# The first MLP product by Strassen's scheme, in groups of six tiles

## The reference

```python
attn = softmax(mask(q @ k^T / 8)) @ v          # 4 x 8 heads, 576 x 64, window of 64
x = attn as (2304, 512)
x[do] = x[do] + gate * (relu(x[do] @ w1[e]) @ w2[e])   # MoE: one of 8 experts for each row that computes
h = x @ w_in                                   # (2304, 512) @ (512, 2048)
g = h * clip(h + 3, 0, 6) / 6
out = g @ w_out                                # (2304, 2048) @ (2048, 512)
```

## Time and profile before

| | us |
|---|---|
| median of three runs | 698.57 (698.03 to 699.78) |
| the profiled execution, its own time | 699.17 |
| its span, first to last instruction | 697.6 |
| TensorE busy in it | 659.5 |
| VectorE, ScalarE, GpSimd busy | 251.9, 243.1, 71.9 |

### The profile page before, as it was taken

One profiled execution on the slowest core, in us unless ns is written; L12 is line 12 of the kernel. 1 busy time (PEld: TensorE's weight loads), 2 busy tenths in 40 slices (PEclk: granted clock), 3 DMA queues, 4 the chain that ended last, 5 costly groups with the idle time before them and its releaser, 6 DMA issues.

```text
span 697.6 us, 17145 instructions
## 1 busy us (share of the span) xinstructions
PE 659.5 (95%) x6654; PEld 580.8 (83%) x6654; DVE 251.9 (36%) x810; ACT 243.1 (35%) x571; POOL 71.9 (10%) x122
## 2 busy tenths in 40 slices
PE   5799997679999999899999999999999999999998
PEld 4678886658877887899899989998999899989996
DVE  2568886001111112465442224223422242233222
ACT  3779984011121112465432223222322232223221
POOL 4322564111111111000000000000000000000000
PEclk9999998899999999999999999999999999999999
DMA  9767879788486176453220002000200020001001
GB/s 171 148 151 194 218 210 388 239 307 292 156 304 219 36 274 194 140 169 121 91 91 0 1 2 90 0 0 0 90 0 0 0 90 0 0 0 47 0 1 45
DMA packets 97155, 78.13 MB, mean 112 GB/s; under 512 B 61697, under 2 KB 76805, under 8 KB 97104
## 3 DMA queue, kind: packets, MB, share of 16 engines
q1 hardware_dynamic: 81632, 44.88, 23.6%
q10 hardware_dynamic: 12496, 26.24, 11.0%
q0 software_dynamic: 2976, 6.32, 2.7%
HBM read 63.23 MB, written 17.52 MB: 116 GB/s over the span
## 4 chain that ended last, share of the span: by engine, by line
PE 81%; DMA 7%; DVE 4%; SPq 3%; ACT 2%; issue 2%; POOLq 0%; DVEq 0%; ACTq 0%
PE bank L844 29%; PE bank L857 19%; PE av L857 10%; PE av L818 7%; PE bank L806 6%; DMA xin<-x_rows 6%; PE bank L619 2%; PE av L663 2%; DVE sm L1081 2%; SPq L412 2%; PE bank L679 2%; PE bank L604 1%; PE av L775 1%; ACT pr L903 1%; PE av L829 1%
## 5 line engine op out<-in xcount | busy, mean ns | idle before, releaser
L1027 ACT ACTIVATE rel<-bank,half 128x384 f32<-128x384 f32 x96 | 55.8, 582 | 185.5 <-PE bank L844 185.5
L1279 DVE SCALAR_TENSOR_TENSOR act<-rel,bank 128x384 f32<-128x384 f32 x96 | 53.2, 554 | 170.1 <-ACT rel L1027 170.1
L844 PE MATMUL bank<-xT_hi,wi_hi 128*128 128x384 f32 x384 | 83.3, 338 | 0.7 <-ACT xT_hi L1020 0.7
L844 PE MATMUL bank<-xT_hi,wi_lo 128*128 128x384 f32 x384 | 82.8, 336 | 0.0
L844 PE MATMUL bank<-xT_lo,wi_hi 128*128 128x384 f32 x384 | 82.0, 334 | 0.0
L1283 DVE TENSOR_TENSOR g_lo<-act,g_hi 128x384 fp32r<-128x384 f32 x96 | 53.6, 558 | 66.8 <-ACT g_hi L1038 66.8
L857 PE MATMUL bank<-wo_hi,g_lo 128*128 128x512 f32 x192 | 76.1, 397 | 0.0
L857 PE MATMUL bank<-wo_hi,g_hi 128*128 128x512 f32 x192 | 76.0, 396 | 0.0
L857 PE MATMUL bank<-wo_lo,g_hi 128*128 128x512 f32 x192 | 75.7, 394 | 0.0
L844 PEld LDWEIGHTS bank<-xT_hi,wi_hi 128*128 128x128 f32 x384 | 68.9, 188 | 7.7 <-ACT xT_hi L1020 0.9
L1038 ACT CAST g_hi<-act 128x384 fp32r<-128x384 f32 x96 | 49.3, 513 | 64.8 <-DVE act L1279 64.8
(11 more groups left out here) (139 smaller groups left out, 794.4 us busy)
## 6 DMA issues: line engine op xcount, KB each, us to landing
w2s<-in_moe_w ACTq DMA_DIRECT2D x7, 2048.0 KB, 10.9
w1s<-in_moe_w ACTq DMA_DIRECT2D x5, 2048.0 KB, 15.9
qraw<-in_q SPq DMA_DIRECT2D x36, 128.0 KB
vnow<-in_v SPq DMA_DIRECT2D x36, 128.0 KB, 3.4
x_new<-xall SPq DMA_DIRECT2D x18, 256.0 KB
out<-ot SPq DMA_DIRECT2D x18, 256.0 KB, 2.1
kraw<-in_k SPq DMA_DIRECT2D x34, 128.0 KB
xn<-x_new SPq DMA_DIRECT2D x17, 256.0 KB, 3.3
```

Source lines behind the costliest of these rows:

```text
L844: last = pe.matmul(bank[f % 4][:, 0:GN], a[:, f, c, :], b[:, c, :], start=(n == 0), stop=(n == 3 * DC - 1))
L1027: sc.activation(rel[f % 2][:, :], bank[f % 4][:, 0:GN], ACT.Relu, scale=1.0 / 6.0, bias=half[:, :]).then_inc(s_rel, 1)
L1279: dve.scalar_tensor_tensor(out=act[f % 2][:, :], in0=rel[f % 2][:, :], scalar=1.0, in1=bank[f % 4][:, 0:GN], op0=ALU.min, op1=ALU.mult).th ...
```

## The change

Six tiles form a group (three groups), and two units form a pair (eight pairs). For a group and a pair, the first product is a 2 by 2 by 2 block product: the 512 inputs are halved (`k`), the six tiles are halved (`t`), and the pair has two units (`u`). Strassen's scheme (in a form with 7 products) computes the four blocks of h from seven products of sums of quarters instead of eight products of quarters.

- **x**: for each group, ScalarE copies the six turned tiles to `xr`. VectorE (three) and GpSimd (two) form five sums or differences of quarters in the buffers `xd[0]` and `xd[1]`, and two quarters are used as they are. ScalarE rounds each of the seven (`x_high`), and VectorE takes the rest (`x_low`).
- **weights**: they are no longer kept. For each group and pair SyncE loads a piece of each weight, GpSimd forms five sums (`combine_w`), and ScalarE and VectorE split them (`w_high`, `w_sums_high`, `w_low`, `o_high`, `o_low`).
- **products**: `product(it, j)` is 6 matmuls of 384 columns into bank 6 or 7 by turns. ScalarE copies products 0 to 4 to SBUF (`mc`). GpSimd forms two blocks of h and two part sums (`hq`, `tsum`, `usum`). VectorE adds products 5 and 6 to the part sums from PSUM. Then relu, act, g_hi and g_lo as before, with two of the four g_lo on GpSimd.
- **second product**: its 36 matmuls for six tiles and two units stand between the products of the next iteration, into banks 0 to 5. The next group's tiles are turned at the end of the iterations 1 to 6 of a group.

The buffers move too: `xc_hi`, `xc_lo`, `xr`, `rel` and `act` lie where the experts' weights were, and the first group's tiles 3 to 5 are loaded into the buffers `ot`. The loops of the MLP are written out in full and no longer run as device loops.

The diff, cut to the parts above:

```diff
-    GN = GT * P
-    NRAW = 4
+    MT = 6
+    MG = NT // MT
+    FP = FC2 // 2
+    NQ = MG * FP
+    GN = MT // 2 * P
+    XQ = DC // 2
...
+        PIECES = ((0, 0), (0, 1)), ((0, 2), (1, 0)), ((1, 1), (1, 2)), ((2, 0), (2, 1)), ((2, 2), (3, 0)), ((3, 1),), ((3, 2),)
+        def m_bank(j):
+            return bank[6 + j % 2]
...
+        def turned(it):
+            G, p = it // FP + 1, it % FP
+            return (G, p - 1) if G < MG and 1 <= p <= MT else None
...
+            def load_w_in(it):
+                if it >= 2:
+                    sp.wait_ge(s_wlo, it - 1)
...
+                for u in range(2):
+                    for h in range(2):
+                        sp.dma_start(wir[it % 2][:, 1 - u + 2 * h, :, :], quarters[:, u, it % FP, h, :, :]).then_inc(s_wir[it % 2], 16)
...
+            def combine_w(it):
+                w, lot = wir[it % 2], wcm
+                pool.wait_ge(s_wir[it % 2], 64 * (it // 2 + 1))
+                if it:
+                    pool.wait_ge(s_wlo, it)
+                pool.tensor_tensor(lot[:, 0:2, :, :], w[:, 0:2, :, :], w[:, 2:4, :, :], ALU.add)
+                pool.tensor_tensor(lot[:, 2:4, :, :], w[:, 0:4:3, :, :], w[:, 1:3, :, :], ALU.subtract)
+                pool.tensor_tensor(lot[:, 4, :, :], w[:, 1, :, :], w[:, 2, :, :], ALU.add).then_inc(s_wcm, 1)
...
+            combine_w(0)
+            combine_x(0, 4)
+            combine_x(0, 6)
+            for it in range(NQ):
+                last_pair = it % FP == FP - 1 and it + 1 < NQ
+                if it + 1 < NQ:
+                    combine_w(it + 1)
+                pool.wait_ge(s_hq, 5 * it + 2)
+                if it:
+                    pool.wait_ge(s_act, 4 * it - 3)
+                pool.tensor_tensor(hq[0][:, :], mc[0][:, :], mc[1][:, :], ALU.add).then_inc(s_cp, 1)
+                pool.wait_ge(s_hq, 5 * it + 3)
+                if it:
+                    pool.wait_ge(s_mc, 2 * it - 1)
+                pool.tensor_tensor(tsum[:, :], mc[1][:, :], mc[2][:, :], ALU.subtract).then_inc(s_cp, 1)
+                if last_pair:
+                    combine_x(it // FP + 1, 4)
+                pool.wait_ge(s_hq, 5 * it + 4)
+                if it:
+                    pool.wait_ge(s_act, 4 * it - 2)
+                pool.tensor_tensor(hq[1][:, :], mc[3][:, :], mc[2][:, :], ALU.add).then_inc(s_cp, 1)
+                if it:
+                    pool.wait_ge(s_mc, 2 * it)
+                pool.tensor_tensor(usum[:, :], mc[3][:, :], mc[0][:, :], ALU.subtract).then_inc(s_cp, 1)
+                low(it, 0)
+                pool.wait_ge(s_hq, 5 * it + 5)
+                pool.wait_ge(s_cp, 6 * it + 4)
+                pool.tensor_tensor(tsum[:, :], tsum[:, :], mc[4][:, :], ALU.add).then_inc(s_cp, 1)
+                pool.tensor_tensor(usum[:, :], usum[:, :], mc[4][:, :], ALU.add).then_inc(s_cp, 1)
+                low(it, 1)
+                if last_pair:
+                    combine_x(it // FP + 1, 6)
...
+            def product(it, j):
+                G, p = it // FP, it % FP
+                if j == 0:
+                    pe.wait_ge(s_wlo, it + 1)
+                    if it:
+                        pe.wait_ge(s_mc, 2 * it)
+                elif j == 1:
+                    if it and turned(it - 1):
+                        pe.wait_ge(s_xr, turned(it - 1)[0] * MT + turned(it - 1)[1] + 1)
+                else:
+                    pe.wait_ge(s_hq, 5 * it + j - 1)
+                if p == 0:
+                    pe.wait_ge(s_xhi, 7 * G + j + 1)
                 n = 0
-                for a, b in ((wi_hi, xT_hi), (wi_lo, xT_hi), (wi_hi, xT_lo)):
-                    if f == 0 and b is xT_lo:
-                        pe.wait_ge(s_mlo, G * GT + GT)
-                        if not isinstance(G, int):
-                            fixed(pe)
-                    for c in range(DC):
-                        last = pe.matmul(bank[f % 4][:, 0:GN], a[:, f, c, :], b[:, c, :],
-                                         start=(n == 0), stop=(n == 3 * DC - 1))
+                for a, b in ((w_hi, xc_hi), (w_lo, xc_hi), (w_hi, xc_lo)):
+                    if p == 0 and b is xc_lo:
+                        pe.wait_ge(s_xlo, 7 * G + j + 1)
+                    for c in range(XQ):
+                        last = pe.matmul(m_bank(j)[:, 0:GN], a[it % 2][:, WSLOT[j], c, :], b[:, j, c, :],
+                                         start=(n == 0), stop=(n == 3 * XQ - 1))
                         n += 1
-                last.then_inc(s_mh, 1)
-
-            def second_product(G, f):
-                pe.wait_ge(s_glo, G * FC2 + f + 1)
-                if isinstance(G, int) and G == 0:
-                    pe.wait_ge(s_wlo, pieces.index(("out", f)) + 1)
-                for i in range(GT):
-                    if f == 0 and not (isinstance(G, int) and G == 0):
-                        pe.wait_ge(s_oc, G * GT - GT + i + 1)
-                    for n, (a, b) in enumerate(((g_hi, wo_hi), (g_hi, wo_lo), (g_lo, wo_hi))):
-                        last = pe.matmul(bank[4 + i][:, :], a[f % 4][:, i * P:(i + 1) * P],
-                                         b[:, f, :],
-                                         start=(f == 0 and n == 0), stop=(f == FC2 - 1 and n == 2))
-                    if f == FC2 - 1:
-                        last.then_inc(s_sum, 1)
-                if f < FC2 - 1:
+                last.then_inc(s_m, 1)
...
+            for it in range(NQ):
+                for j in range(7):
+                    product(it, j)
+                    for c, i in PIECES[j]:
+                        if it:
+                            second_product(it - 1, c, i)
+                if turned(it):
+                    transpose_tile(*turned(it))
+            for c in range(4):
+                for i in range(3):
+                    second_product(NQ - 1, c, i)
...
+            w_high(0)
+            w_sums_high(0)
+            for i in range(3):
                 take_x(0, i)
-            mlp(0)
-            with sc.Fori(1, NG - 1) as G:
-                mlp(G)
-            mlp(NG - 1)
+            x_high(0, 0)
+            x_high(0, 1)
+            for i in range(3, MT):
+                take_x(0, i)
+            for j in range(2, 7):
+                x_high(0, j)
+            for it in range(NQ):
+                G, p = it // FP, it % FP
+                more = it + 1 < NQ
+                nextx = p == FP - 1 and more
+                take_product(it, 0)
+                if it:
+                    high(it - 1, 3)
+                    if turned(it - 1):
+                        take_x(*turned(it - 1))
+                if more:
+                    w_high(it + 1)
+                take_product(it, 1)
+                if nextx:
+                    x_high(G + 1, 0)
+                if more:
+                    w_sums_high(it + 1)
+                take_product(it, 2)
+                if nextx:
+                    x_high(G + 1, 1)
+                relu(it, 0)
+                take_product(it, 3)
+                high(it, 0)
+                if nextx:
+                    x_high(G + 1, 2)
+                o_high(it)
+                relu(it, 1)
+                take_product(it, 4)
+                high(it, 1)
+                if G and p == 0:
+                    for i in range(3):
+                        take_out(G - 1, i)
+                if nextx:
+                    x_high(G + 1, 3)
+                    x_high(G + 1, 4)
+                relu(it, 2)
+                high(it, 2)
+                relu(it, 3)
+                if nextx:
+                    x_high(G + 1, 5)
+                    x_high(G + 1, 6)
...
+            def add_product(it, c):
+                dve.wait_ge(s_m, 7 * it + c + 4)
+                dve.wait_ge(s_cp, 6 * it + c + 3)
+                if it:
+                    dve.wait_ge(s_act, 4 * it + c - 3)
...
+            w_low(0)
+            x_low(0, 0)
+            combine_x(0, 1)
+            x_low(0, 1)
+            x_low(0, 2)
+            combine_x(0, 3)
+            x_low(0, 3)
+            combine_x(0, 5)
+            x_low(0, 4)
+            x_low(0, 5)
+            x_low(0, 6)
+            for it in range(NQ):
+                G, p = it // FP, it % FP
+                more = it + 1 < NQ
+                nextx = p == FP - 1 and more
+                if it:
+                    low(it - 1, 3)
+                if G and p == 0:
+                    x_low(G, 5)
+                    x_low(G, 6)
+                if G and p == 1:
+                    take_out(G - 1, 5)
+                if more:
+                    w_low(it + 1)
+                if nextx:
+                    x_low(G + 1, 0)
+                    combine_x(G + 1, 1)
+                activate(it, 0)
+                if nextx:
+                    x_low(G + 1, 1)
+                    combine_x(G + 1, 3)
+                o_low(it)
+                activate(it, 1)
+                if nextx:
+                    x_low(G + 1, 2)
+                    x_low(G + 1, 3)
```

(49 more changed lines are left out.)

359 lines of the change are left out of this document (207 added, 152 removed).

## The result

The changed kernel takes 784.06 us (780.0 to 785.11, four runs) against 698.3 for the kernel before: 1.121 of its time, interval 1.117 to 1.126. That is 86 us slower. The direction was forecast, the size was not: 752 was predicted, and 784 lies above the range (710 to 775). The profiled execution has a span of 783.4 us.

What follows compares the result with a forecast made beforehand. The prediction took the MLP before the change as bound by TensorE, matmuls without a gap. Start 315.5, iterations 402, changes of group 22, last matmuls 8.3 and tail 3.5 gave a 751 us span, 752 us time, range 710 to 775.

Steps and rivals of the forecast that it cites:

- 402 and 22 us: Main loop with holds: 402 us for iterations 1 to 23 as common ones, 22 us extra for the two changes of group.
- Mutual hold: MLP loop: VectorE and GpSimd each block the other while reading SBUF; span 751 us, chance 0.55.
- The start gains 1.5 us of it, each change of group 3: Extra time put for the hold outside common iterations: 1.5 us at the start, 3 us at each change of group.
- The unheld part of the changes: Preparing the next group's x in iterations 7 and 15 and the following ones: 8.2 us a change without holds, 16.4 in all.
- The start: Before iteration 1: first x and weight sums and product copies, to 312.0 us, plus 2 for low clock; 315.5 with the hold.
- the 0.25 us taken off each iteration for overlap: Iterations 1 to 23: instructions issued back to back overlap, taking 0.25 us off each and 408 us down to 402.
- the 0.82 us for 384 columns on GpSimd: GpSimd's two-input sums in the MLP: assumed 0.82 us at 384 columns, between 0.50 and 1.0.
- Nobody's reads matter: Rival for the MLP: no SBUF hold, or GpSimd arithmetic doesn't hold VectorE; span 717 us, chance 0.14.
- only VectorE is held: Rival for the MLP: GpSimd's reads hold VectorE but not the reverse, 0.3 to 0.5 us an iteration; span 726, chance 0.13.
- Not slower: Rival: TensorE never waits in the loop, decided by an average wait below 0.3 us an iteration; 691 us, chance 0.10.
- Worse: Rival: GpSimd takes 1.0 us each with both engines holding, 1.3 us more an iteration; 781 us, chance 0.08.
- the 25.2 us: First product in the MLP: 42 matmuls instead of 48, saving 1.05 us in each of 24 iterations, 25.2 us in all.

Runs made afterwards that it cites:

- run 7: Changed kernel with all GpSimd MLP arithmetic on VectorE and the orders mended (start, turned tile, first quarter difference, weight sums, output copy): 714.92 us, ratio 1.025.
- Run 1: Changed kernel with each two-input GpSimd instruction in the MLP replaced by two constant fills, so GpSimd reads nothing from SBUF: 718.17 us, ratio 1.032.
- run 4: Changed kernel with VectorE's first output copy of a group moved behind act 3, from in front of the add of product 6: 781.16 us, ratio 1.119.
- run 2: Changed kernel with all of GpSimd's MLP arithmetic done by VectorE, nothing left out: 728.97 us, ratio 1.044.
- run 9: As run 7, but without the quarters of x, their sums and splitting for the second and third group: 696.02 us, ratio 0.998.
- Run 5: Changed kernel with the six matmuls of product 3 done twice, so 48 matmuls an iteration again: 803.61 us, ratio 1.154.
- run 8: As run 7, but with the three weight-sum instructions on GpSimd again: 731.39 us, ratio 1.051.
- run 10: Kernel before the change, plus 240 GpSimd subtractions of 384 columns on an SBUF tile the MLP does not use: 707.29 us, ratio 1.013.

## Why the prediction was right and wrong

The forecast's 402 and 22 us are regrouped here: 332 for the 19 iterations outside the changes of group (ten with a turned tile at 18.15 us, nine without at 16.75), and 92 for the four inside (7, 8, 15 and 16: the same common times and the 22 us of the changes). Then the forecast span is 315.5 + 332 + 92 + 11.8 = 751 us, and the measured one 316.1 + 349 + 107.6 + 10.7 = 783 us. Of the 32 us that were missing, 17 lie outside the changes and 16 inside; the end was 1 us shorter. (The transposes were put at 0.43 us each, where 68.25 - 66.9 us for three gives 0.45; run 7 shows 0.42.)

**Right: the mechanism.** Mutual hold was the likeliest case, and both timelines show it. The working gave 18.4 us with a tile and 17.0 without, and the trace has 18.60 and 17.39. The copy of the turned tile, which product 1 waits for, was put at 3.7 us of the iteration and ends at 3.55.

**Wrong: "The start gains 1.5 us of it, each change of group 3".** This is the step that failed, in both halves. I had worked the held timetable through for a common iteration only and guessed it for the rest. A change of group was to take 8.2 + 3 = 11.2 us over two common iterations, and took 19.0 and 16.6. Run 1, where nothing is held, has 11.9 and 7.5 over its own common ones. So the hold adds 7.1 and 9.1 us to a change, beyond what it adds to any two iterations, where 3 was put: 10 us of the missing 32. There both engines work on 768 columns, and each long instruction waits for the other's. VectorE's difference of 0.95 us and GpSimd's sum of 1.80, side by side:

```profile
438.84 2.55 POOL L661 TENSOR_TENSOR xd<-xr 128x768 f32<-128x768 f32 x1
...
439.61 2.59 DVE L1486 TENSOR_TENSOR xd<-xr 128x768 f32<-128x768 f32 x1
```

ScalarE stands in order behind that difference for 5.2 us (2.8 in run 1), and with it relu 0 and the copy of product 3.

The unheld part of the changes, 8.2 us each, was put 3 us too low for the two together. What was left out there is the store in front of the add, which no term had. It costs 3.7 us in run 4, and it is no part of the hold: run 1, without GpSimd's reads, has it in iteration 8 as well, and takes 23.06 us there against 18.65 in 16.

```profile
443.90 5.76 DMA out<-ot
```

**The start: right in its sum by luck.** Iteration 1 was put at 315.5 us and starts at 316.15, and product 2 at 301.35 and starts at 301.06. But from the first product to iteration 1 the hold costs 7.0 us and not 1.5 (30.3 us against 23.3 in run 1, 24.7 in run 2). This did not show, since the start without it had been put 3.5 us too long (26.8 us), and the first product came 1.4 us early. So the 717 us for the case without holds, which run 1 meets with a span of 716.0, is luck too: there iteration 1 starts at 306.8 us instead of 314, and the 23 iterations take 6 us more than was put.

**Too small: the iterations outside the changes, 17 us.** The common iterations account for ten of these 17 us: 18.15 and 16.75 us were used, against 18.60 and 17.39. Two terms of that sum are open to doubt, and no run parts them: the 0.25 us taken off each iteration for overlap, and the 0.82 us for 384 columns on GpSimd, where this kernel's sums take 0.99 alone, the upper bound of the text. Besides, relu from SBUF takes 0.62 us, in run 1 too, and not the 0.58 that it was left at. The other 6.5 us are iterations 1, 9 and 17, which were put as common ones and take 20.05, 19.70 and 18.95 us. In the first two TensorE's clock was low for a part (columns as in the earlier trace rows):

```profile
316.15:336.20 20.05, 19.00 (x83) 16.85 (x83) 11.31 (x12) 9.10 (x17) 13.36 (x12) 0.86 0.27 80
484.17:503.87 19.70, 18.65 (x82) 16.50 (x83) 10.87 (x14) 9.09 (x17) 10.28 (x9) 0.87 0.32 103
```

The forecast had the low clock at the start alone, where it was granted 0.68 from 286 to 320 us. It came at each change as well, during and after TensorE's waits. What it costs there no run shows.

**The rivals.** "Nobody's reads matter" and "only VectorE is held" are refuted by the two timelines. "Not slower" put the point at 0.3 us of wait per iteration, and the changed kernel has 1.7 to 2.5; run 9's span of 694.6 us shows that its sum (691) was some 4 us too low even with every hold gone and the changes nearly free. "Worse" (781 us, chance 0.08) comes nearest to the measured span, and its premise holds, 1.0 us for each of GpSimd's sums. But its price does not: it put 1.3 us more on every iteration, and the common ones have 0.2 and 0.4 more than the 18.4 and 17.0. The missing time was elsewhere, so the 781 is near by luck. In none of the traces does an engine wait in the MLP for the load of a weight.

**Where the 25.2 us went.** Run 5 shows that 19.5 of them were gained. The start takes 30 us instead of 7.35. From the changed kernel to run 7, 69 us are holds and orders; from run 7 to run 9, 19 us are the changes of group; what is left is the saved matmuls against a start of 24 us and the waits and low clock near it.

## What to carry to other kernels

Count what VectorE and GpSimd each read from SBUF before giving GpSimd a share: here a VectorE instruction with both inputs in SBUF and a GpSimd instruction that reads SBUF ran one after the other (run 8 against run 7, and both timelines), so the share is no gain unless one of them has slack or takes an input from PSUM. Here moving 11 us of GpSimd work an iteration (its length unheld) onto VectorE saved 55 us in all. A scheme that trades matmuls for sums pays only if the sums and their splits fit beside the matmuls at the borders of the loop too: work out the first iteration and the change of group instruction by instruction, with the holds in it, as they cost more here than 24 iterations gained.

## What was not expected of the hardware

GpSimd's two-input float32 arithmetic in the changed kernel took 0.71 us at 256 columns, 0.99 at 384, 1.26 at 512 and 1.80 at 768, the shortest of each: 0.17 us and 2.13 ns a column, against 0.82 ns for its copies. That is not the price of every such instruction: the subtractions of run 10, whose inputs and output are one tile, took 0.83 us at 384 columns, and no run shows what makes the difference. Beside such a stream a single VectorE instruction waits for one of GpSimd's and then gets its turn (1310 ns instead of 686 in run 10), so neither engine shuts the other out.
